# Gated linear attention and two FFN layers on one core: weight splits, ELU and zero products in the opening

## What is computed

```python
# attention: batch 4, 8 heads, 768 tokens, head dimension 48
f = 1 / (1 + exp(-f_logit))
for t in range(S):
    state = f[t, :, None] * state + outer(k[t], v[t])
    y[t] = q[t] @ state
x = y as (3072 tokens, 384)
# first FFN layer, w_in 384 x 2048, w_out 2048 x 384, ELU
h = x @ w_in
x = where(h > 0, h, exp(min(h, 0)) - 1) @ w_out
# second FFN layer, same sizes, squared ReLU
out = square(max(x @ w_in, 0)) @ w_out
```

## Time and profile before

| | us |
|---|---|
| median of 3 runs | 1005.48 (1005.15 to 1005.61) |
| the profiled execution | 1005.5 |
| its span, first to last instruction | 1003.7 |
| TensorE busy | 966.9 (96%) |
| DVE busy | 534.9 (53%) |
| ACT busy | 390.6 (39%) |
| POOL busy | 302.3 (30%) |
| mean granted TensorE clock | 0.991 |

### The profile page before, as it was taken

How to read it: one execution, slowest core, us unless ns; L and a number is a source line. 1 busy time by engine, 2 the same in 40 slices (tenths; PEclk the granted TensorE clock), 3 DMA queues, 4 the chain that set the end, 5 groups by cost and what they waited for, 6 DMA issues and landing times.

```text
span 1003.7 us, 27605 instructions
## 1 busy us (share of the span) xinstructions
PE 966.9 (96%) x11972; PEld 823.4 (82%) x11972; DVE 534.9 (53%) x758; ACT 390.6 (39%) x685; POOL 302.3 (30%) x243
## 2 busy tenths in 40 slices
PE   5888888999999999999999999999999999999998
PEld 4777766888888888878787879999999999999997
DVE  5679595676767686766425663333333333333332
ACT  3436542434543443443435443232242332322322
POOL 4547573544545363535332542000000000000000
PEclk9989998999999999999999999999999999999999
DMA  8244323221320313022002322000010010000000
GB/s 262 57 138 123 107 65 96 67 64 39 92 77 22 97 35 96 24 56 71 11 2 95 98 83 72 1 32 32 1 63 0 19 44 0 31 31 0 32 1 31
DMA packets 54187, 56.88 MB, mean 57 GB/s; under 512 B 19520, under 2 KB 46400, under 8 KB 54080
## 3 DMA queue, kind: packets, MB, share of 16 engines
q1 hardware_dynamic: 51376, 44.12, 15.3%
q10 hardware_dynamic: 2704, 11.17, 3.1%
HBM read 45.84 MB, written 9.44 MB: 55 GB/s over the span
## 4 chain that ended last, share of the span: by engine, by line
PE 89%; DVE 4%; issue 3%; ACT 2%; DMA 1%; POOL 0%; SPq 0%; DVEq 0%; POOLq 0%; ACTq 0%
PE ps L1531 8%; PE ps L1530 8%; PE ps L1535 8%; PE ps L1569 7%; PE ps L1568 7%; PE ps L1572 7%; PE ps L1068 6%; PE ps L1180 6%; PE ps L1203 5%; PE ps L1182 5%; PE ps L1189 5%; PE ps L1205 5%; PE ps L1209 5%; PE ps L1130 2%; PE ps L1085 1%
## 5 line engine op out<-in xcount | busy, mean ns | idle before, releaser
L1484 DVE TENSOR_TENSOR g<-g 128x512 f32<-128x512 f32 x96 | 66.8, 696 | 263.9 <-ACT g L1404 263.9
L666 POOL TENSOR_TENSOR glo<-g,ghi 128x512 fp32r<-128x512 f32 x80 | 109.5, 1369 | 235.9 <-ACT ghi L489 235.9
L1404 ACT ACTIVATE g<-ps 128x512 f32<-128x512 f32 x112 | 66.9, 598 | 284.7 <-PE ps L1535 280.4
L1530 PE MATMUL ps<-xhi,wts 128*128 128x512 f32 x336 | 131.9, 393 | 0.7 <-ACT xhi L474 0.7
L1531 PE MATMUL ps<-xhi,wts 128*128 128x512 f32 x336 | 131.9, 393 | 0.0
L1569 PE MATMUL ps<-wts,ghi 128*128 128x384 f32 x380 | 128.9, 339 | 0.0
L1568 PE MATMUL ps<-wts,ghi 128*128 128x384 f32 x380 | 127.6, 336 | 0.0
L482 ACT ACTIVATE e<-ps 128x512 f32<-128x512 f32 x80 | 47.7, 596 | 153.3 <-PE ps L1189 153.2
L1180 PE MATMUL ps<-xhi,wts 128*128 128x512 f32 x240 | 99.0, 413 | 2.1 <-ACT g L483 1.3
L1203 PE MATMUL ps<-ghi,wts 128*128 128x512 f32 x234 | 95.8, 409 | 3.4 <-ACT ghi L489 3.4
L873 DVE TENSOR_SCALAR e<-e 128x512 f32<-128x512 f32 x80 | 45.7, 571 | 96.1 <-ACT e L482 95.9
(11 more groups left out here) (118 smaller groups left out, 1664.4 us busy)
## 6 DMA issues: line engine op xcount, KB each, us to landing
raw<-w SPq DMA_DIRECT2D x64, 192.0 KB, 2.4
q<-qk SPq DMA_DIRECT2D x22, 256.0 KB, 4.0
gate<-fl SPq DMA_DIRECT2D x10, 512.0 KB, 5.3
k<-qk SPq DMA_DIRECT2D x10, 512.0 KB, 3.7
x<-xo ACTq DMA_DIRECT2D x6, 768.0 KB, 3.4
xs<-x ACTq DMA_DIRECT2D x6, 768.0 KB, 4.3
out<-PT SPq DMA_DIRECT2D x24, 192.0 KB, 1.9
v<-vn SPq DMA_DIRECT2D x11, 384.0 KB, 3.5
```

The source lines that it names most:

```text
L666: nc.gpsimd.tensor_tensor(out=glo[:, f % 2, :], in0=g[:, f % 2, :], in1=ghi[:, f % 2, :].bitcast(F32), op=ALU.subtract).then_inc(s_glo, 1)
L1530: nc.tensor.matmul(h, w(0, k), xhi[:, k, :], start=(k == 0), stop=False)
```

## The change

Three parts.

Weights: 16 chunks instead of 4 are split before FFN tile 0. The first twelve are loaded into a buffer of their own (`stage`), which shares its memory with xhi, xlo, ghi and glo that are written only later; ACT waits for their twelve low parts before it writes the first xhi. Chunks 12 to 15 go through `raw`. The other 16 follow after slices 0, 2, 4 (two each), 8, 10 (four each) and 11 (two). DVE makes all low parts, POOL none. SP's loads move accordingly.

ELU: `activate` is one SCALAR_TENSOR_TENSOR, min(exp(h) - 1, relu(h)), which equals ELU on both sides of zero.

TensorE: seven products of zeros (the cleared state, 256 columns) at the start instead of two of 384, and one ahead of each product of levels 1 to 6 and each key transposition of units 0 and 1. They write a part of the PSUM pair that nothing reads, after the wait for the pair and ahead of the wait for q and k, which moves behind the other waits there. POOL clears the state before PT. The level 1 product of unit (1, 0) moves ahead of hidden slice 1, and DVE takes its level 1 copy ahead of ELU 1. The second half of the first gates is issued by ACT, not by SP.

```diff
--- before.py
+++ after.py
@@ -36,12 +36,13 @@
 ACC = 4
 HID = 7
 
-FIRST_SPLIT = 4
+FIRST_SPLIT = 16
+STAGED = 12
 
 
 def split_at(c, f):
 
-    return [i for i in (2 * f + 4, 2 * f + 5) if c == 1 and i < 2 * NF]
+    return {0: range(16, 18), 2: range(18, 20), 4: range(20, 22), 8: range(22, 26), 10: range(26, 30), 11: range(30, 32)}.get(f, ()) if c == 1 else ()
...
-        xhi, xlo = sb("xhi", [P, KD, TOK], F32R), sb("xlo", [P, KD, TOK], F32R)
         e = sb("e", [P, 2, TOK])
         g = sb("g", [P, 2, TOK])
+        with nc.sbuf_tensor("stage", [P, STAGED, DM], F32) as stage:
+            pass
+        xhi, xlo = sb("xhi", [P, KD, TOK], F32R), sb("xlo", [P, KD, TOK], F32R)
...
+    def w1_raw(i):
+        return stage[:, i, :] if i < STAGED else raw[:, i % 4, :]
+
+    def w1_loaded(i):
+        return (s_raw[i], 16) if i < STAGED else (s_raw[STAGED + i % 4], (i - STAGED) // 4 * 16 + 16)
...
-        def load_half(c, h, u):
-
-            sp.dma_start(keys_of(c, h)[:, u * W:(u + 1) * W], qk[c * B + 2 * h + u, :, W:2 * W]).then_inc(s_k_in[h % 2], 16)
-            sp.dma_start(gate[:, h % 2, u * W:(u + 1) * W], fl[c * B + 2 * h + u, :, :]).then_inc(s_f[h % 2], 16)
-
         def load_weights(chunks):
             for i in chunks:
-                if i >= 4:
+                if i >= STAGED + 4:
                     sp.wait_ge(s_wlo[i % 2], (i - 4) // 2 + 1)
-                sp.dma_start(raw[:, i % 4, :], w1[chunk_at(i), :, :]).then_inc(s_raw[i % 4], 16)
-
-        def load_weights_beside(c, f):
-
-            load_weights(i + 4 for i in split_at(c, f) if i + 4 < 2 * NF)
+                sp.dma_start(w1_raw(i), w1[chunk_at(i), :, :]).then_inc(w1_loaded(i)[0], 16)
...
         def first_period():
-            load_weights_beside(1, 0)
             sp.wait_ge(*level(s_mm, 1, 0, 1))
             load_padded_v(1, 0)
-            load_weights_beside(1, 1)
+            load_weights(range(18, 20))
             sp.wait_ge(*level(s_mm, 1, 0, 2))
             load_v(1, 0)
-            load_weights_beside(1, 2)
+            load_weights(range(20, 22))
             sp.wait_ge(*level(s_mm, 1, 0, 3))
             load_gates(1, 2)
-            load_weights_beside(1, 3)
+            load_weights(range(22, 24))
             sp.wait_ge(*level(s_mm, 1, 1, 0))
             load_padded_v(1, 1)
-            load_weights_beside(1, 4)
             sp.wait_ge(*level(s_mm, 1, 1, 1))
             load_gates(1, 3)
-            for f in range(5, 8):
-                load_weights_beside(1, f)
+            load_weights(range(24, 26))
 
...
         def second_period():
             load_k(1, 2)
-            load_weights_beside(1, 8)
             load_q(1, 2)
             load_v(1, 1)
-            load_weights_beside(1, 9)
+            load_weights(range(26, 30))
             sp.wait_ge(*level(s_mm, 1, 2, 0))
             load_padded_v(1, 2)
-            for f in range(10, 16):
-                load_weights_beside(1, f)
+            load_weights(range(30, 32))
             load_k(1, 3)
             load_v(1, 2)
             load_q(1, 3)
...
         load_q(0, 0)
-        load_half(0, 0, 1)
+        sp.dma_start(keys_of(0, 0)[:, W:2 * W], qk[1, :, W:2 * W]).then_inc(s_k_in[0], 16)
         load_q(0, 1)
         sp.dma_start(ident[:], ident_d).then_inc(s_ident, 16)
         sp.wait_ge(s_zero, 4)
         load_padded_v(0, 0)
         load_v(0, 0)
-        load_weights(range(2))
+        load_weights(range(4))
         load_gates(1, 0)
-        load_weights(range(2, FIRST_SPLIT))
+        load_weights(range(4, 8))
         load_gates(1, 1)
+        load_weights(range(8, 12))
         load_q(1, 0)
         sp.wait_ge(*level(s_mm, 0, 1, 2))
         load_k(1, 0)
         load_padded_v(0, 1)
         load_v(0, 1)
+        load_weights(range(12, 16))
         sp.wait_ge(s_last, 2)
-        load_weights(range(FIRST_SPLIT, FIRST_SPLIT + 4))
+        load_weights(range(16, 18))
         load_q(1, 1)
         load_k(1, 1)
         first_period()
@@ -413,7 +410,7 @@
...
         def split_weights(chunks):
             for i in chunks:
-                act.wait_ge(s_raw[i % 4], (i // 4 + 1) * 16)
-                nc.scalar.activation(wts[:, chunk_at(i), 0, :], raw[:, i % 4, :], ACT.Copy).then_inc(s_whi, 1)
+                act.wait_ge(*w1_loaded(i))
+                nc.scalar.activation(wts[:, chunk_at(i), 0, :], w1_raw(i), ACT.Copy).then_inc(s_whi, 1)
...
             take5(1, 0)
-            split_weights(split_at(1, 5))
             hidden_copies(1, 6)
...
-            split_weights(split_at(1, 9))
             ffn_step(10)
...
-            split_weights(split_at(1, 13))
...
         act.dma_start(keys_of(0, 0)[:, 0:W], qk[0, :, W:2 * W]).then_inc(s_k_in[0], 16)
-        act.dma_start(gate[:, 0, 0:W], fl[0, :, :]).then_inc(s_f[0], 16)
+        for u in range(UB):
+            act.dma_start(gate[:, 0, u * W:(u + 1) * W], fl[u, :, :]).then_inc(s_f[0], 16)
...
-        split_weights(range(2))
+        split_weights(range(4))
         gates(1, 0, True)
-        split_weights(range(2, FIRST_SPLIT))
+        split_weights(range(4, 8))
         gates(1, 1, True)
         nc.scalar.activation(warm[:, 1:2], warm[:, 0:1], ACT.Exp)
+        split_weights(range(8, 12))
         take4(0, 0)
         take4(0, 1)
...
         krow_copy(0, 1)
+        split_weights(range(12, FIRST_SPLIT))
+        for i in range(2):
+            act.wait_ge(s_wlo[i], STAGED // 2)
         first_x_split()
         first_period()
...
         nc.gpsimd.memset(q[:, :, :, 0:1], 0.0)
         nc.gpsimd.memset(queries(0, 0)[:, :, 0:1], 0.0).then_inc(s_zero, 1)
+        nc.gpsimd.memset(state[:, :, :], 0.0).then_inc(s_zero, 1)
         nc.gpsimd.memset(PT[:, :, 0:2 * X, :], 0.0).then_inc(s_zero, 1)
-        nc.gpsimd.memset(state[:, :, :], 0.0).then_inc(s_zero, 1)
         nc.gpsimd.memset(vz[:, :, :, :, D:P - D], 0.0).then_inc(s_zero, 1)
...
-        def split_weights(chunks):
-            for i in chunks:
-                if i % 2:
-                    continue
-                n = chunk_at(i)
-                pool.wait_ge(s_whi, i + 1)
-                nc.gpsimd.tensor_tensor(out=wts[:, n, 1, :], in0=raw[:, i % 4, :],
-                                        in1=wts[:, n, 0, :].bitcast(F32), op=ALU.subtract).then_inc(s_wlo[0], 1)
...
         def first_period():
-            ffn_step(0)
+            low(1, 0)
             k_update(1, 0, 1)
-            ffn_step(1)
+            low(1, 1)
             k_update(1, 0, 2)
-            ffn_step(2)
+            low(1, 2)
             k_update(1, 0, 3)
-            ffn_step(3)
+            low(1, 3)
             k_update(1, 0, 4)
...
-        split_weights(range(FIRST_SPLIT))
         keep_last(1, 0)
         k_update(1, 0, 0)
...
             else:
-                dve.wait_ge(s_zero, 3)
+                dve.wait_ge(s_zero, 2)
...
         def split_weights(chunks):
             for i in chunks:
-                if i % 2 == 0:
-                    continue
                 n = chunk_at(i)
                 dve.wait_ge(s_whi, i + 1)
-                nc.vector.tensor_tensor(out=wts[:, n, 1, :], in0=raw[:, i % 4, :],
-                                        in1=wts[:, n, 0, :].bitcast(F32), op=ALU.subtract).then_inc(s_wlo[1], 1)
+                nc.vector.tensor_tensor(out=wts[:, n, 1, :], in0=w1_raw(i),
+                                        in1=wts[:, n, 0, :].bitcast(F32), op=ALU.subtract).then_inc(s_wlo[i % 2], 1)
...
         def activate(c, f):
 
             dve.wait_ge(s_e, nth(c, f + 1))
-            es, gs = e[:, f % 2, :], g[:, f % 2, :]
-            nc.vector.tensor_scalar(es, es, 1.0, -1.0, ALU.min, ALU.add).then_inc(s_m, 1)
-            dve.wait_ge(s_m, nth(c, f + 1))
             dve.wait_ge(s_r, nth(c, f + 1))
-            nc.vector.tensor_tensor(out=gs, in0=gs, in1=es, op=ALU.add).then_inc(s_g, 1)
+            nc.vector.scalar_tensor_tensor(out=g[:, f % 2, :], in0=e[:, f % 2, :], scalar=-1.0, in1=g[:, f % 2, :],
+                                           op0=ALU.add, op1=ALU.min).then_inc(s_g, 1)
...
         def first_period():
             ffn_step(0)
             q_update(1, 0, 1)
+            rest(1, 0, 1)
             activate(1, 1)
-            rest(1, 0, 1)
-            split_weights(split_at(1, 1))
             q_update(1, 0, 2)
...
-        split_weights(range(FIRST_SPLIT))
+        split_weights(range(12))
         state_update(0, 0)
         state_update(0, 1)
+        split_weights(range(12, FIRST_SPLIT))
         first_x_split()
         step(1, 0, 0)
...
     @blk.tensor
     def _(pe):
+        def keep_warm(n, banks):
+
+            for _ in range(n):
+                nc.tensor.matmul(banks[:, 0, 256:512], state[:, 1, 0:P], state[:, 0, 0:256], start=True, stop=True)
+
         def product(c, h, l):
 
             if l == 0:
@@ -1022,9 +997,6 @@
                     pe.wait_ge(s_ys, count(c, h, 1, -3))
                 elif past(c, h, 3):
                     pe.wait_ge(*taken(c, h - 1, EARLY))
-            else:
```

(79 more changed lines are left out.)

## The result

The changed kernel takes 1000.18 us (median of 4 runs, 999.58 to 1000.9) against 1005.55 us before: ratio 0.9941, interval 0.9927 to 0.9955. It is 0.6% faster, by 5.4 us of the medians, where 12.6 were forecast; 1000.2 lies above the forecast range of 987 to 999.

The account below looks back on a forecast made before the run. TensorE is busy nearly throughout from 172 us, so all gain lies before. 2.0 (opening) + 9.7 (waits, moved product) - 0.8 (new wait) + 1.7 (clock) = 12.6 us; 1005.5 - 12.6 = 992.9, about 993; range 987 to 999.

Parts of the forecast that it names:

- Zeros: Opening, before 54.2 us: zeros fit into TensorE's idle time at no cost; shorter products at 2.4 GHz win 2.0 us.
- the zeros lift nothing in the levels: Rival, chance 0.12: in the opening the clock stays at 1.2 GHz, 4.0 us lost instead of 2.0 won; time 999.
- The reading of the Trainium skill weighed there: Opening levels: already at the full clock rate, so the zeros would bring nothing; sum 10.6, time 995.
- Loads: Opening: eight more loads of 192 KB push back the next unit's gates, which nobody wants before 54 us; cost nothing.
- Twelve splits on DVE: Before the first state products: 7.5 us of splits, 5.6 new against 6.59 free; cost nothing, 2 us if cover is gone.
- The exclusion with POOL: Opening: two-SBUF-input DVE operations and GpSimd ones exclude each other; three key updates could lose 1.6 us; left out of sum.
- The rest: Stage B, 54.2 to 172 us: fewer TensorE waits win 9.7 us, less 0.8 for a new wait, plus 1.7 of clock.
- the lower clock near 130 us: Behind tile 10's output: with the wait before it gone, the lower clock should not come; 1.7 us won.
- The wait put at 0.8 for the high part 11: Late in stage B: four splits stand on DVE ahead of ELU 11; a new wait of 0.8 us.
- the move: Stage B: product level 1 ahead of hidden tile 1 fills its 1.3 us wait for ACT's relu; 1.1 us won.
- Beyond 160 us: The 3.2 us wait for q at 162 us and its lower clock stay untouched.
- a rival: More clock, chance 0.15: one or both kept low-clock stretches, 3.4 us each, vanish; time 988.

Follow-up runs that it names:

- the small zeros: 14 zero products of 64 columns in TensorE's wait for q: changed kernel without zeros between, loads later, old chunk order, 995.96 us; same without zeros between, early loads, 996.8 us.

## Why the prediction was wrong, step by step

**Zeros, the step that failed.** The prediction put the zeros at nothing, "into what is free", and took 2.0 us won in the opening, on the ground that the clock would be at 2.4 GHz. It was there for the first product only: the lower clock came with the 3.4 us wait for q of unit 1, and 14 zeros between products did not lift it. At 1.2 GHz a zero took 1.15 us from start to start (0.97 was worked out), 16.1 us for the 14, against the 5.6 us idle that the prediction had counted. It stood ahead of each wait, so a product whose q and k had come stayed behind it. DVE, full before, then waited for TensorE (busy 21.45 of 24.80 us for 24.24). Measured in place of the 2.0 won: 8.3 us of opening lost on the kernel before, 5.2 in the changed one. The rival "the zeros lift nothing in the levels" had the mechanism and its outer price, 8.0; its middle, 4.0 with half hidden by DVE, was too kind, and a chance of 0.12 too small: the row that spoke for it, TensorE busy 19.16 of 24.80 at the low rate, was the only evidence on the question. That its 999 us comes near the measured 1000.2 is luck: it put 4.0 lost and 10.6 won, where 9.2 were lost and 13.8 won. The reading of the Trainium skill weighed there (the levels at the full rate already) is refuted by more than the transposes now: TensorE was busy 24.80 of 24.80 us at a granted 0.50.

**Loads, the second.** "Nobody wants those before 54 us" was asked of the data only. Eight more loads beside the levels cost the opening 4.1 us on the kernel before, 3.8 of them in TensorE's waits for instructions, and some 4.0 in the changed one. The prediction held the rows for it, DMA share 0.53 in that stretch and waits marked issue, and took neither for a resource in use.

**Twelve splits on DVE: right.** They took 7.41 us from 43.57 us (7.5 was put), and their place didn't delay the first state products. The exclusion with POOL that the prediction takes from the Trainium skill, "SBUF — State Buffer", the part on the shared port pair, does show, on the other side. The two key updates beside the splits took 1.21 and 1.25 us, no more than in the levels of the kernel before (1.07 to 1.58), but a split that lay beside each took 1.40 us where the others took 0.54. Four splits around the first update:

```profile
L829 DVE TENSOR_TENSOR wts<-stage,wts x4: 544/546/1398, 43.6 to 45.8; 128x384 fp32r<-128x384 f32 x4
```

Each of the two ended 0.4 us behind its update, most of a split's own time, as if it had stood until POOL was done. The 1.7 us lost so (2 x 0.85) fell in DVE's free time and not, as the 1.6 put, on POOL's path.

**The rest: right in size.** To the load of q at the end of y of unit (1, 1) the changed kernel needs 95.3 us from the first hidden tile (158.66 less 63.40), the one before 106.2 (160.34 less 54.16): 10.9 won, 9.7 - 0.8 + 1.7 = 10.6 forecast. TensorE's waits in it fell by 7.7 us (10.5 to 2.8; 8.9 were put), the lower clock near 130 us gave its 1.7, and 1.5 are not traced: the closeness is in part luck. The SCALAR_TENSOR_TENSOR took 0.95 us (0.98 put). The wait put at 0.8 for the high part 11 did not come (0.7 in all, elsewhere). No lower clock near 130 us, as forecast. Of its parts the move, put at 1.1, can't be told from nothing, and the splits won more than ELU.

**Beyond 160 us: 2.9 us more,** 13.8 in all. The wait for q fell from 3.2 to 1.7 us and the clock's low stretch halved, which the prediction had only in a rival. The pauses alone don't give it: with the small zeros the low stretch was halved in one run and not in the other.

Sum: forecast 2.0 + 10.6 = 12.6; measured - 5.2 - 4.0 + 10.9 + 2.9 = 4.6 by the profiled spans, 5.4 by the medians.

## What to carry to other kernels

A filler ahead of a wait is free only if it is shorter than the wait at the clock that it will really have: price it at the lower rate, and look whether the engine that it is to help is the one the others wait for. A load that nothing waits for can still take time, from an engine that runs through many small instructions and waits for their fetch; issue it where fewer of them are left (here eight loads issued from about 32 us on cost 0.8 us in place of 4.1). Cut a change in parts before it is kept: here the opening lost nine microseconds to the zeros and the time of the loads, while the splits and ELU behind it won eleven.

## What the runs showed of the hardware that was not expected

- TensorE stayed at 1.2 GHz from about 13.5 to 49 us while it was busy without a gap, on zero products of 128x128 by 256 columns and products of 48 rows in turn; it rose within the transposes. Brought in at 2.4 GHz, it fell at about 18 us all the same, whether zeros stood between the products or not.
- TensorE waits for its instructions in small matmuls. The waits come every 128 matmul records and end 1.2 to 1.6 us behind a 16384 byte packet of the queue marked instruction. They last 0.2 to 2.9 us, 1.3 us in all from 10 to 46 us of the kernel before, 5.1 beside eight more loads. They move by as many records as are put ahead of them: 28 records took 2.5 us of them away near 150 us and brought 6 us more in the opening, and the time stayed where it was (995.56 and 995.96).
- A DVE subtraction of 128x384 with two inputs in SBUF took 0.54 us alone and 1.40 when POOL's update of 128x512 lay across it.
